# Attention with a position bias and two dense layers on one core: three tiles of head 1 scored ahead of head 0's last tile

## The chip, the cores and the metric

The kernel runs on one core of a Trainium2 chip. The metric is the device time of one execution in microseconds, the median of three runs.

## The reference, cut to what matters

```python
# q, k, v: (4, 8, 576, 64); 8 heads in each of 4 batches
scores = q @ k.T / 8
rel = |i - j|;  x = log1p(rel) / log1p(max(i, 1))
bias = relu(x * w1 + b1) @ w2            # (576, 576, 8): one table for each head, the same in all batches
attn = softmax(scores + bias);  o = attn @ v
x = o as (2304, 512)
x = (s * relu(x @ w_in)**2 + b) @ w_out  # 512 -> 2048 -> 512
h = x @ w2_in;  out = (h - tanh(h)) @ w2_out
```

All inputs and the output are float32.

## The kernel before

The program has three stages on one core. **The bias stage** builds the bias tables in 36 packs. TensorE makes them, ScalarE and VectorE write them to the tile stage, and SyncE stores each pack to bias_flat in DRAM (line 323). A bias tile (128 rows of one head, 288 KB) is read back from there with skewed rows (sp_bias). A tile can be loaded only when the packs with its rows have landed. For the last tile of head 0 (tile 4, 64 rows, 144 KB) these are all 36 (load_bias, called at line 986).

**The attention stage** runs over 32 heads (head n = batch times 8 plus head) of five row tiles each, so step g is tile t of head n with g = 5n + t. Every engine has its own function for a step, and walks through the same steps g in order. In a step, TensorE scores tile g (pe_score: four matmuls into ps_s or ps_o), VectorE adds the bias and takes the row maximum (line 767), ScalarE takes the exponential and the row sum (line 643). Five steps later, the tile of the head before is turned on TensorE (five transposes, pe_turn), rounded by ScalarE (pth, line 659), its low part is made by VectorE (ptl, line 735), and TensorE multiplies it with v (pe_value). So all matmuls have a high and a low part. The first turn of a head waits for the exponentials of all its tiles (line 590). In steps 5 to 9 the turns of head 0 thus stand beside the scores of head 1.

q and k of a head are rounded on the way: ScalarE rounds q (act_round_q, line 198), GpSimd (POOL) rounds k and makes both low parts (lines 203, 212 and 208). SyncE issues every load in the order of the steps: after VectorE's add of tile t of head n comes bias tile t of head n + 1 (line 798), and with it k (t = 2) and q (t = 4) of head n + 2.

**The dense stage** is 5 units of 64 blocks of matmuls. After 49 steps of attention alone, the other steps of attention are placed between its blocks. Its first two weight blocks are rounded by ScalarE and their low parts made by POOL after step 3 (lines 1032 and 1014).

The order is written out by hand: it is that of the loops at the end, and semaphores do the rest (s_done, min_done, exp_done and others count tiles in the order in which their engine does them).

Of the kernel before, what the change touches and what calls it, by code (L numbers as in the profile page):

```python
# [12 lines left out]
P = 128  # L13
DMA = 16
# [6 lines left out]
HIDS = 2  # L21
LATE = 2
EXTRA = 3
TURNED = 10
PLANE = 2.0 ** -15
RING = 4
# [4 lines left out]
def build(nc, qt, kt, vt, net, w2s, psi, lam, lam_rows, sb, w1, w2, w3, w4, out):  # L31
# [41 lines left out]
    def scoring(n):  # L73

        return n < BH
# [9 lines left out]
    with ExitStack() as ctx:  # L85
# [108 lines left out]

        def act_round_q(act, n):
            act.wait_ge(q_loaded, (n + 1) * DMA)
            need(act, s_done, (n - 1) * NT)
            act.activation(q2[:, n % 2, 0:S], q_raw[:], ACT.Copy, scale=lower[:, 0:1]).then_inc(q_hi_done, 1)  # L198

        def pool_round_k(pool, n):  # L200
            pool.wait_ge(k_loaded, (n + 1) * DMA)
            need(pool, s_done, (n - 1) * NT)
            pool.tensor_copy(k2h[:, n % 2, :], k_raw[:]).then_inc(k_hi_done, 1)

        def pool_low_q(pool, n):
# [18 lines left out]
            pass  # L224
        planes = tile("planes", [P, 2, 2 * S], F16)
        o_tmp = tile("o_tmp", [D, 2, HALF])
        neg_max = tile("neg_max", [P, NT])
        den = tile("den", [P, 2, NT])
        den_e = tile("den_e", [P, NT])
        inv = tile("inv", [P, NT])  # L230
# [205 lines left out]
        def slot(i):  # L436

            return i % 2

        def score_bank(n, t):  # L440

            if n == 0 and t % 2:
                return ps_o
            return ps_t if n > TURNED and (n * NT + t) % 2 else ps_s

        FIRST_PLANE = TURNED * NT
# [119 lines left out]
        def pe_score(pe, n, t):  # L566
            if t == 0:
                pe.wait_ge(q_lo_done, n + 1)
                pe.wait_ge(k_lo_done, n + 1)
            if n == 0:  # L570
                need(pe, min_done, t - 1)
                pe.wait_ge(back_done, PACKS - 2 if t == 0 else PACKS)
            elif n <= TURNED:
                pe.wait_ge(min_done, n * NT + t)
            else:
                if n == TURNED + 1 and t == 0:
                    pe.wait_ge(pt_lo_done, FIRST_PLANE)
                pe.wait_ge(p_lo_done, n * NT + t - FIRST_PLANE - 1)
            for half in range(2):
                cols = slice(half * HALF, (half + 1) * HALF)  # L580
                acc = score_bank(n, t)[:, half, 0:HALF]
                lhs = q2[:, n % 2, P * t:P * (t + 1)]
                pe.matmul(acc, lhs, k2h[:, n % 2, cols], start=True, stop=False)  # L583
                mm = pe.matmul(acc, lhs, k2l[:, n % 2, cols], start=False, stop=True)  # L584
            mm.then_inc(s_done, 1)

        def pe_turn(pe, i, alone):
            v, t = divmod(i, NT)
            if t == 0:
                pe.wait_ge(exp_done, (v + 1) * NT)  # L590
            need(pe, pt_lo_done, i - alone)
            R = ROWS[t]
            acc = turn_bank(i, alone)
            for r in range(NT):
                mm = pe.transpose(acc[0:R, P * r:P * (r + 1)], p_t[:, v % 2, r, P * t:P * t + R], ident[:])
            mm.then_inc(pt_done, 1)
# [7 lines left out]
        def pe_step(pe, g, alone):  # L604

            n, t = divmod(g, NT)
            value = pe_value if (valued(g) or 0) < FIRST_PLANE else pe_value_planes
            if t == 3 and turning(n):
                pe_turn_inv(pe, n - 1)
            if scoring(n):  # L610
                pe_score(pe, n, t)
            if valued(g) is not None and t != 2:
                value(pe, valued(g))
            if turned(g) is not None:
                pe_turn(pe, turned(g), alone)
            if valued(g) is not None and t == 2:
                value(pe, valued(g))
# [9 lines left out]
        def act_plane(act, f):  # L627
# [3 lines left out]
            act.activation(halves(plane(f)[:, 0:S]), score_home(n, t), ACT.Copy, scale=inv_n[:, t:t + 1])\  # L631
                .then_inc(p_hi_done, 1)

        def act_step(act, g, alone, between=None):
            n, t = divmod(g, NT)
            i, j = turned(g), valued(g)

            def exponential():
                if t == 0:
                    need(act, den_done, min(n - 1, TURNED))  # L640
                act.wait_ge(min_done, g + 1)
                p = score_home(n, t)
                act.activation(p, p, ACT.Exp, scale=-1.0, bias=neg_max[:, t:t + 1],
                               accum_out=den[:, n % 2, t:t + 1]).then_inc(exp_done, 1)
# [8 lines left out]
            if scoring(n) and alone and t == NT - 1:  # L653
                exponential()
# [8 lines left out]
            if scoring(n) and not (alone and t == NT - 1):  # L663
                exponential()
            if n >= TURNED and between:
                between()
            if TURNED <= n < BH:
                act.wait_ge(exp_done, g + 1)
                act.activation(sum_n[:, t:t + 1], den[:, n % 2, t:t + 1], ACT.Copy, scale=PLANE, bias=1e-9 * PLANE)\
                    .then_inc(sum_done, 1)  # L670
            if t == 0 and turning(n):
                v = n - 1
                need(act, inv_done, v)
                act.wait_ge(exp_done, (v + 1) * NT)
                act.activation(den_e[:], den[:, v % 2, :], ACT.Copy, bias=1e-9).then_inc(den_done, 1)
            if t == 1 and n + 1 < BH:
                act_round_q(act, n + 1)

        def pool_step(pool, g):
# [10 lines left out]
            if t == 1 and n >= 2 and n % 2 == 1 and n - 2 < TURNED:  # L690
                pool_scale(pool, n - 2)
                if n == H + 1:
                    pool_split(pool, KD - 1)
            if t == 1 and n + 1 < BH:
                pool_low_q(pool, n + 1)
            if t == 3 and scoring(n):
                pool.wait_ge(v_loaded, (n + 1) * DMA)
# [45 lines left out]
        def dve_plane(dve, f):  # L743
# [3 lines left out]
                                     in1=halves(plane(f)[:, 0:S]), op0=ALU.mult, op1=ALU.subtract)\  # L747
                .then_inc(p_lo_done, 1)

        def dve_step(dve, g, alone, between=None):  # L750
# [5 lines left out]
            if scoring(n):  # L756
                dve.wait_ge(s_done, g + 1)
# [5 lines left out]
            if scoring(n):  # L763
                dve.wait_ge(bias_loaded[t], (n + 1) * DMA)
                if t == 0 and n < TURNED:
                    need(dve, pt_done, (n - 1) * NT)
                dve.tensor_tensor_reduce(out=score_home(n, t), in0=score_bank(n, t)[:, :, 0:HALF],  # L767
                                         in1=halves(bias_t[:, t, :]), scale=-SCALE, scalar=3.0e38,
                                         op0=ALU.add, op1=ALU.min, accum_out=neg_max[:, t:t + 1])\
                    .then_inc(min_done, 1)  # L770
            if f is not None:
                dve_plane(dve, f)
            if i is not None:
# [16 lines left out]
        def sp_step(sp, g):  # L790
# [3 lines left out]
                sp.wait_ge(inv_row_done, v + 1)  # L794
                sp.dma_start(inv_rows[v, :].rearrange("(t p) -> t p", p=P), inv_row[:]).then_inc(inv_stored, DMA)
            if n + 1 < BH:
                sp.wait_ge(min_done, n * NT + t + 1)
                sp_bias(sp, n + 1, t)
            f = planes_of(g)
            if f is not None:  # L800
# [182 lines left out]
        @block.sync  # L983
        def _(sp):
            sp_biases(sp)
            load_bias(sp, NT - 1)
            for g in STEPS_AT[:FIRST]:
                sp_step(sp, g)
                n, t = divmod(g, NT)
                if t == 2 and n in (3, 5, 7):  # L990
                    sp_weights(sp, (n - 1) // 2)
# [35 lines left out]
        def _(act):  # L1027
            act_biases(act)
            act.wait_ge(sb_loaded, DMA)
            for g in STEPS_AT[:FIRST]:  # L1030
                act_step(act, g, True)
                if g == 3:
                    act_weights(act, 0)
                    act_weights(act, 1)
                if g == H * NT:
                    act_weights(act, 2)
# [7 lines left out]
        def _(dve):  # L1044
            dve_biases(dve)
            dve.wait_ge(sb_loaded, DMA)
            for g in STEPS_AT[:FIRST]:
                dve_step(dve, g, True)
            dve_low(dve, turned(FIRST - 1), True)
            for u in range(NU):  # L1050
# [6 lines left out]
        def _(pe):  # L1057
            pe_biases(pe)
            pe.wait_ge(ident_done, 1)
            pe.wait_ge(q_clear, 2)  # L1060
            for g in STEPS_AT[:FIRST]:
                pe_step(pe, g, True)
            pe.wait_ge(pt_lo_done, turned(FIRST - 1))
            for u in range(NU):
# [67 lines left out]
```

## Time and profile before

| | us |
|---|---|
| median of 3 runs | 1096.89 (1096.28 to 1096.93) |
| the profiled execution | 1097.03 |
| its span | 1095.2 |
| TensorE busy | 1049.5 |
| ScalarE busy | 728.6 |
| POOL busy | 681.7 |
| VectorE busy | 619.1 |

The span runs from the first to the last instruction of the program on the core; the rest of the time lies outside it. TensorE (PE in the rows, PEld for its weight loads) is busy for 96% of the span. DVE is VectorE, ACT is ScalarE, SP is SyncE and SPq its queue of transfers. The busy time of matmuls is modelled, and rows of neighbouring instructions overlap a little.

### The profile page before, as it was taken

Reading aid. Unit: us, or ns where it says so; the run is one execution under the profiler, and the core shown is the slowest. Engines: PE = TensorE matmul, PEld = TensorE weight load, DVE = VectorE, ACT = ScalarE, POOL = GpSimd, SP = SyncE. Lnnn points to the kernel's source line nnn. Section 1 sums busy time; section 2 is a strip of 40 time slices with the busy share of each in tenths; the row PEclk is TensorE's granted clock in tenths of the full one; section 3 lists DMA queues with packets and bytes.
Section 4 is the critical chain, followed back from the end, with each engine's and each line's share of the span. In section 5 each row is a group of like instructions: output and inputs, shape, how many; then the busy total and the mean of one; then the engine's idle time right before and its main releaser. Section 6 shows DMA issues by size and latency. Waiting matters only on the chain.

```text
span 1095.2 us, 16840 instructions
## 1 busy us (share of the span) xinstructions
PE 1049.5 (96%) x5668; PEld 910.9 (83%) x5668; DVE 619.1 (57%) x1128; ACT 728.6 (67%) x1469; POOL 681.7 (62%) x656
## 2 busy tenths in 40 slices
PE   5679999999999999999999999999999999999998
PEld 1158889888888888888888888888888888999998
DVE  7968877745765476567646754761450461450640
ACT  8968878866877677778767876873562563553652
POOL 1045675687778678777786787765554555455453
PEclk9989999999999999999999999999999999999999
DMA  5778876798889788998896799664333233333331
GB/s 177 256 242 273 269 225 173 194 253 239 189 218 258 215 188 234 240 214 207 242 268 169 185 255 270 171 160 131 113 98 114 96 115 124 111 129 99 97 122 63
DMA packets 185480, 202.48 MB, mean 185 GB/s; under 512 B 125954, under 2 KB 128692, under 8 KB 185396
## 3 DMA queue, kind: packets, MB, share of 16 engines
q1 hardware_dynamic: 185108, 201.35, 66.7%
q8 instruction: 45, 0.74, 0.3%
q14 instruction: 39, 0.32, 0.1%
q10 hardware_dynamic: 288, 0.07, 0.0%
HBM read 156.55 MB, written 15.64 MB: 157 GB/s over the span
## 4 chain that ended last, share of the span: by engine, by line
PE 70%; ACT 10%; issue 6%; POOL 5%; DMA 4%; DVE 4%; SPq 1%; DVEq 0%; ACTq 0%; POOLq 0%
PE ps_f L906 20%; PE ps_f L908 20%; PE ps_f L907 20%; PE ps_o L544 2%; POOL wl L863 2%; ACT x_raw L342 2%; DVE g_buf L966 2%; PE ps_s L583 2%; ACT gh L919 2%; PE ps_o L547 2%; PE ps_s L584 1%; DMA bias_flat<-stage 1%; ACT stage L359 1%; POOL pth L689 1%; ACT planes L631 1%
## 5 line engine op out<-in xcount | busy, mean ns | idle before, releaser
L863 POOL TENSOR_TENSOR wl<-w_raw,wh 128x512 fp32r<-128x512 f32 x318 | 417.5, 1318 | 282.6 <-ACT wh L856 282.1
L906 PE MATMUL ps_f<-gh,wh 128*128 128x464 f32 (+1 forms) x640 | 242.6, 379 | 1.7 <-DVE g_buf L966 1.7
L906 PE MATMUL ps_f<-xh,wh 128*128 128x464 f32 (+1 forms) x640 | 240.5, 376 | 0.6 <-DVE ptl L735 0.6
L908 PE MATMUL ps_f<-xh,wl 128*128 128x464 f32 (+1 forms) x640 | 237.4, 371 | 0.0
L907 PE MATMUL ps_f<-gl,wh 128*128 128x464 f32 (+1 forms) x640 | 237.4, 371 | 0.0
L908 PE MATMUL ps_f<-gh,wl 128*128 128x464 f32 (+1 forms) x640 | 237.2, 371 | 0.0
L907 PE MATMUL ps_f<-xl,wh 128*128 128x464 f32 (+1 forms) x640 | 237.1, 371 | 0.0
L856 ACT ACTIVATE wh<-w_raw 128x512 fp32r<-128x512 f32 x318 | 196.4, 623 | 48.8 <-PE ps_f L908 48.6
L906 PEld LDWEIGHTS ps_f<-gh,wh 128*128 128x128 f32 x640 | 120.8, 189 | 14.9 <-DVE g_buf L966 2.8
L906 PEld LDWEIGHTS ps_f<-xh,wh 128*128 128x128 f32 x640 | 120.5, 188 | 13.4 <-DVE ptl L735 0.8
L908 PEld LDWEIGHTS ps_f<-xh,wl 128*128 128x128 f32 x640 | 120.1, 188 | 13.4
L908 PEld LDWEIGHTS ps_f<-gh,wl 128*128 128x128 f32 x640 | 120.1, 188 | 13.0
L907 PEld LDWEIGHTS ps_f<-xl,wh 128*128 128x128 f32 x640 | 120.2, 188 | 12.8
L907 PEld LDWEIGHTS ps_f<-gl,wh 128*128 128x128 f32 x640 | 120.2, 188 | 11.8
L929 ACT ACTIVATE r_buf<-ps_f 128x464 f32<-128x464 f32 (+1 forms) x160 | 88.1, 551 | 58.9 <-PE ps_f L908 58.1
L957 DVE TENSOR_TENSOR gl<-g_buf,gh 128x464 fp32r<-128x464 f32 (+1 forms) x80 | 81.3, 1016 | 47.6 <-ACT gh L923 47.6
L954 DVE SCALAR_TENSOR_TENSOR gl<-g_buf,sb_c,gh 128x464 fp32r<-128x464 f32 (+1 forms) x80 | 73.8, 922 | 53.0 <-ACT gh L919 53.0
L966 DVE SCALAR_TENSOR_TENSOR g_buf<-ps_f,sb_c,r_buf 128x464 f32<-128x464 f32 (+1 forms) x80 | 55.4, 693 | 41.8 <-ACT r_buf L929 40.4
L689 POOL CAST pth<-p_t 128x576 fp32r<-128x576 f16 x110 | 77.7, 706 | 0.0
L208 POOL TENSOR_TENSOR q<-q_raw,q 128x576 fp32r<-128x576 f32 x32 | 45.8, 1432 | 44.8 <-ACT q L198 42.3
L583 PE MATMUL ps_s<-k2h,q 128*128 128x288 f32 x210 | 65.3, 325 | 6.5 <-DVE neg_max L767 6.1
L919 ACT ACTIVATE gh<-g_buf,sb_c 128x464 fp32r<-128x464 f32 (+1 forms) x80 | 54.3, 678 | 21.0 <-DVE g_buf L966 21.0
(124 smaller groups left out, 1688.7 us busy)
## 6 DMA issues: line engine op xcount, KB each, us to landing
w_raw<-in_w_out SPq DMA_DIRECT2D x80, 512.0 KB, 3.7
w_raw<-in_w_in SPq DMA_DIRECT2D x79, 512.0 KB, 3.5
bias_t<-bias_flat SPq DMA_DIRECT2D x128, 288.0 KB, 4.0
bias_flat<-stage SPq DMA_DIRECT2D x36, 295.5 KB, 2.3
k_raw<-in_kt SPq DMA_DIRECT2D x32, 288.0 KB, 4.2
q_raw<-in_qt SPq DMA_DIRECT2D x32, 288.0 KB, 3.3
v_raw<-in_vt SPq DMA_DIRECT2D x32, 288.0 KB, 3.4
bias_t<-bias_flat SPq DMA_DIRECT2D x32, 144.0 KB, 3.9
```

Of the source, the lines that this page charges most:

```text
L583: pe.matmul(acc, lhs, k2h[:, n % 2, cols], start=True, stop=False)
L689: pool.tensor_copy(pth[:, slot(i), :], turned_planes(i // NT)[:, i % NT, :]).then_inc(block_cast, 1)
L856: act.activation(wh[:, b % RING, :, :], raw_block(b), ACT.Copy)\
L863: pool.tensor_tensor(wl[:, b % RING, :, :], raw_block(b), wh[:, b % RING, :, :].bitcast(F32), ALU.subtract).then_inc(w_lo_done, 1)
L906: pe.matmul(acc, hi, rhs_h[:, k0 + kk, 0:T], start=(first and kk == 0), stop=False)
L907: pe.matmul(acc, hi, rhs_l[:, k0 + kk, 0:T], start=False, stop=False)
L908: mm = pe.matmul(acc, lo, rhs_h[:, k0 + kk, 0:T], start=False, stop=(last and kk == 3))
L919: act.activation(gh[:, j, 0:T], g_buf[:, n % 2, 0:T], ACT.Identity, bias=sb_c[:, 1:2])\
L929: act.activation(r_buf[:, n % 2, 0:T], acc, (ACT.Relu, ACT.Tanh)[l]).then_inc(r_done, 1)
L954: dve.scalar_tensor_tensor(out=gl[:, j, 0:T], in0=g_buf[:, n % 2, 0:T], scalar=sb_c[:, 1:2], in1=hi, op0=ALU.add, op1=ALU.subtract).then_i ...
L957: dve.tensor_tensor(gl[:, j, 0:T], g_buf[:, n % 2, 0:T], hi, ALU.subtract)\
L966: dve.scalar_tensor_tensor(out=g_buf[:, n % 2, 0:T], in0=acc, scalar=sb_c[:, 0:1], in1=r, op0=ALU.mult, op1=ALU.mult).then_inc(g_done, 1)
```

## The change

Three tiles of head 1 (PRE = 3, steps 5 to 7) are scored, biased and exponentiated ahead of the last tile of head 0 (step 4). Their steps keep the other work. scored_ahead(g) is the place of tile g in the new order, all_scored(n) the number of tiles scored when head n is complete. The score banks go on to alternate between ps_s and ps_o through the eight tiles. SyncE issues the last bias load of head 0 after its steps 0 to 2. ScalarE rounds q of head 1 right behind the bias stage, before the first exponential, and POOL makes its low part in step 0. The rounding of the first two weight blocks on ScalarE comes after step 4, no longer after step 3. The row maxima have two sets, for even and odd heads.

```diff
+PRE = 3
 def act_round_q(act, n):
     act.wait_ge(q_loaded, (n + 1) * DMA)
-    need(act, s_done, (n - 1) * NT)
+    need(act, s_done, all_scored(n - 2) if n > 1 else 0)
...
-neg_max = tile("neg_max", [P, NT])
+neg_max = tile("neg_max", [P, 2, NT])
...
+def scored_ahead(g):
+    if NT <= g < NT + PRE:
+        return g - 1
+    return NT + PRE - 1 if g == NT - 1 else g
+def all_scored(n):
+    return NT + PRE if n == 0 else (n + 1) * NT
+def scoring_at(g):
+    return g < TILES and not NT <= g < NT + PRE
 def score_bank(n, t):
-    if n == 0 and t % 2:
-        return ps_o
+    if n * NT + t < NT + PRE:
+        return ps_o if scored_ahead(n * NT + t) % 2 else ps_s
...
 # pe_score
-if n == 0:
-    need(pe, min_done, t - 1)
+if n * NT + t < NT + PRE:
+    need(pe, min_done, scored_ahead(n * NT + t) - 1)
...
 # pe_turn, first tile of head v
-pe.wait_ge(exp_done, (v + 1) * NT)
+pe.wait_ge(exp_done, all_scored(v))
...
 # act_step
-if t == 1 and n + 1 < BH:
+if t == 1 and 0 < n < BH - 1:
     act_round_q(act, n + 1)
 # pool_step
-if t == 1 and n + 1 < BH:
+if t == (1 if n else 0) and n + 1 < BH:
     pool_low_q(pool, n + 1)
 # sp_step
-sp.wait_ge(min_done, n * NT + t + 1)
+sp.wait_ge(min_done, scored_ahead(g) + 1)
 sp_bias(sp, n + 1, t)
...
 # SyncE
-load_bias(sp, NT - 1)
 for g in STEPS_AT[:FIRST]:
+    if g == PRE:
+        load_bias(sp, NT - 1)
     sp_step(sp, g)
...
 # ScalarE
+act_round_q(act, 1)
 for g in STEPS_AT[:FIRST]:
+    if g == NT - 1:
+        for pre in range(NT, NT + PRE):
+            act_exp(act, pre)
     act_step(act, g, True)
-    if g == 3:
+    if g == NT - 1:
         act_weights(act, 0)
         act_weights(act, 1)
...
 # VectorE, before step NT - 1
+        for pre in range(NT, NT + PRE):
+            dve_add(dve, pre)
 # TensorE, before step NT - 1
+        for pre in range(NT, NT + PRE):
+            pe_score(pe, *divmod(pre, NT))
```

act_exp and dve_add are the exponential and the add of one tile, with the lines that act_step and dve_step held before.

On SyncE, at the end of the bias stage, before (bias_flat<-stage are the last two stores, the 64-row load is head 0's last tile, the three of 128 rows are head 1's):

```order
L323 DMA bias_flat<-stage 128x591 [waits back_done] x2
L218 DMA bias_t<-bias_flat 64x576 [waits stage_stored3,stage_stored2,bias_clear,stage_stored1,stage_stored0]
L218 DMA bias_t<-bias_flat 128x576 [waits min_done] x3
L188 DMA k_raw<-in_kt 128x576 [waits k_lo_done]
L218 DMA bias_t<-bias_flat 128x576 [waits min_done]
```

and now:

```order
L324 DMA bias_flat<-stage 128x591 [waits back_done] x2
L219 DMA bias_t<-bias_flat 128x576 [waits min_done] x3
L189 DMA k_raw<-in_kt 128x576 [waits k_lo_done]
L219 DMA bias_t<-bias_flat 64x576 [waits stage_stored3,stage_stored2,bias_clear,stage_stored1,stage_stored0]
L219 DMA bias_t<-bias_flat 128x576 [waits min_done]
```

The three loads of head 1 and k of head 2 moved ahead of head 0's last tile and its wait for the stores.

On ScalarE, from the end of the bias stage to the turned tile 0 of head 0 (p_t,den is an exponential, q a rounding of q, wh one of a weight block), before:

```order
L643 ACTIVATE p_t,den<-p_t,neg_max 128x576 [waits min_done]
L198 ACTIVATE q<-q_raw,lower 128x576 [waits q_loaded]
L643 ACTIVATE p_t,den<-p_t,neg_max 128x576 [waits min_done] x2
L856 ACTIVATE wh<-r_buf 128x512 [waits w_first]
L856 ACTIVATE wh<-g_buf 128x512 [waits w_first]
L643 ACTIVATE p_t,den<-p_t,neg_max 128x576 [waits min_done]
L659 ACTIVATE pth<-ps_f 128x576 [waits pt_done]
```

and now:

```order
L199 ACTIVATE q<-q_raw,lower 128x576 [waits q_loaded,sb_loaded]
L655 ACTIVATE p_t,den<-p_t,neg_max 128x576 [waits min_done] x8
L876 ACTIVATE wh<-r_buf 128x512 [waits w_first]
L876 ACTIVATE wh<-g_buf 128x512 [waits w_first]
L674 ACTIVATE pth<-ps_f 128x576 [waits pt_done]
```

The rounding of q moved to the front, eight exponentials stand in a row, and the two weight roundings stand between the last of them and the turned tile.

## Rows read from the trace of the kernel before

**Rows 1.** The page: busy time, share of the span, instructions of each engine.

```profile
PE 1049.5 (96%) x5668; PEld 910.9 (83%) x5668; DVE 619.1 (57%) x1128; ACT 728.6 (67%) x1469; POOL 681.7 (62%) x656
```

**Rows 2.** The chain that ended last, 64 to 71.6 us: start us, us, what.

```profile
61.15 5.21 DMA bias_flat<-stage
...
66.49 2.92 DMA bias_t<-bias_flat
...
69.54 0.76 DVE p_t L767
```

**Rows 3.** Timeline of TensorE: start us, us, instruction, count, idle before it.

```profile
70.45 0.58 PE L583 MATMUL ps_s<-k2h,q 128*128 128x288 f32 x1 [6.15 <-DVE neg_max L767]
...
75.73 0.71 PE L595 MATMUL ps_f<-ident,p_t 128*128 128x128 f32 x5
...
76.86 0.38 PE L583 MATMUL ps_s<-k2h,q 128*128 128x288 f32 x1
...
80.45 0.38 PE L583 MATMUL ps_s<-k2h,q 128*128 128x288 f32 x1
```

**Rows 4.** Stretches: length, busy by engine, granted clock, DMA share, GB/s.

```profile
67.00:68.00 1.00, 0.00 (x0) 0.00 (x0) 0.00 (x0) 0.00 (x0) 1.00 (x2) 1.00 0.22 35
68.00:69.00 1.00, 0.00 (x0) 0.00 (x0) 0.00 (x0) 0.00 (x0) 1.00 (x2) 0.82 0.81 228
69.00:70.00 1.00, 0.00 (x0) 0.00 (x0) 0.46 (x1) 0.00 (x0) 0.60 (x1) 0.50 0.98 350
75.00:76.00 1.00, 1.00 (x8) 1.00 (x8) 0.58 (x3) 0.96 (x2) 1.00 (x1) 0.77 0.73 207
```

**Rows 5.** Timeline of ScalarE.

```profile
61.88 0.78 ACT L643 ACTIVATE p_t<-p_t,neg_max 128x576 f32<-128x576 f32 x1 [1.74 <-DVE neg_max L767]
...
66.29 0.61 ACT L856 ACTIVATE wh<-g_buf 128x512 fp32r<-128x512 f32 x1
...
71.02 0.18 ACT L643 ACTIVATION_READ_ACCUMULATOR p_t<-p_t,neg_max 128x1 f32 x1
72.86 0.65 ACT L659 ACTIVATE pth<-ps_f 128x576 fp32r<-128x576 f32 x1 [1.65 <-PE ps_f L595]
```

**Rows 6.** Timeline of VectorE.

```profile
61.70 0.09 DVE L767 DVE_READ_ACCUMULATOR2_ANT neg_max<- 128x1 f32 x1
...
63.37 0.08 DVE L767 DVE_READ_ACCUMULATOR2_ANT neg_max<- 128x1 f32 x1
...
74.66 0.75 DVE L735 TENSOR_TENSOR ptl<-ps_f,pth 128x576 fp32r<-128x576 f32 x1
```

**Rows 7.** Timeline of SyncE's queue: first issue, us, count.

```profile
66.49 2.09 SPq L218 DMA_DIRECT2D bias_t<-bias_flat  x4
...
70.83 0.58 SPq L183 DMA_DIRECT2D q_raw<-in_qt  x1
```

**Rows 8.** DMA view, 64 to 67.5 us: 40 slices; packets, MB, share; issues, landing.

```profile
GB/s 0 0 0 0 0 0 0 27 0 0 27 0 0 27 0 27 27 27 27 27 0 0 0 0 0 0 0 0 0 0 0 0 0 0 0 0 0 0 0 0
...
q1 hardware_dynamic: 9, 0.02, 2.1%
...
bias_t<-bias_flat SPq DMA_DIRECT2D x1, 288.0 KB, 3.1
```

**Rows 9.** DMA view, 61 to 67 us: packets, MB, share of 16 engines.

```profile
q8 instruction: 1, 0.02, 1.9%
```

**Rows 10.** DMA view, 62 to 63 us.

```profile
DMA packets 195, 0.42 MB, mean 420 GB/s; under 512 B 23, under 2 KB 23, under 8 KB 194
```

**Rows 11.** Timeline of POOL.

```profile
67.12 1.26 POOL L863 TENSOR_TENSOR wl<-r_buf,wh 128x512 fp32r<-128x512 f32 x1
...
73.99 0.66 POOL L203 CAST k2h<-k_raw 128x576 fp32r<-128x576 f32 x1 [4.38 <-DMA k_raw<-in_kt]
74.73 1.42 POOL L212 TENSOR_TENSOR k2l<-k_raw,k2h 128x576 fp32r<-128x576 f32 x1
77.20 1.43 POOL L208 TENSOR_TENSOR q<-q_raw,q 128x576 fp32r<-128x576 f32 x1 [1.04 <-ACT q L198]
```

More of the change, by code:

```diff
@@ L201, in pool_round_k @@
             pool.wait_ge(k_loaded, (n + 1) * DMA)
-            need(pool, s_done, (n - 1) * NT)
+            need(pool, s_done, all_scored(n - 2) if n > 1 else 0)
             pool.tensor_copy(k2h[:, n % 2, :], k_raw[:]).then_inc(k_hi_done, 1)
@@ L569, in pe_score @@
                 pe.wait_ge(k_lo_done, n + 1)
-            if n == 0:
-                need(pe, min_done, t - 1)
-                pe.wait_ge(back_done, PACKS - 2 if t == 0 else PACKS)
+            if n * NT + t < NT + PRE:
+                need(pe, min_done, scored_ahead(n * NT + t) - 1)
+                pe.wait_ge(back_done, PACKS - 2 if n + t == 0 else PACKS)
             elif n <= TURNED:
@@ L609, in pe_step @@
                 pe_turn_inv(pe, n - 1)
-            if scoring(n):
+            if scoring_at(g):
                 pe_score(pe, n, t)
@@ L632, in act_plane, with act_exp @@
                 .then_inc(p_hi_done, 1)
+        def act_exp(act, g):
+            n, t = divmod(g, NT)
+            if t == 0:
+                need(act, den_done, min(n - 1, TURNED))
+            act.wait_ge(min_done, scored_ahead(g) + 1)
+            p = score_home(n, t)
+            act.activation(p, p, ACT.Exp, scale=-1.0, bias=neg_max[:, n % 2, t:t + 1],
+                           accum_out=den[:, n % 2, t:t + 1]).then_inc(exp_done, 1)
         def act_step(act, g, alone, between=None):
@@ L636, in act_step @@
             i, j = turned(g), valued(g)
[L638 to L644, printed above, removed]
             if j is not None and j % NT == NT - 1:
@@ L652, in act_step @@
                 act_plane(act, f)
-            if scoring(n) and alone and t == NT - 1:
-                exponential()
+            if scoring_at(g) and alone and t == NT - 1:
+                act_exp(act, g)
             if i is not None:
@@ L662, in act_step @@
                 between()
-            if scoring(n) and not (alone and t == NT - 1):
-                exponential()
+            if scoring_at(g) and not (alone and t == NT - 1):
+                act_exp(act, g)
             if n >= TURNED and between:
@@ L673, in act_step @@
                 need(act, inv_done, v)
-                act.wait_ge(exp_done, (v + 1) * NT)
+                act.wait_ge(exp_done, all_scored(v))
                 act.activation(den_e[:], den[:, v % 2, :], ACT.Copy, bias=1e-9).then_inc(den_done, 1)
-            if t == 1 and n + 1 < BH:
+            if t == 1 and 0 < n < BH - 1:
                 act_round_q(act, n + 1)
@@ L748, in dve_plane, with dve_add @@
                 .then_inc(p_lo_done, 1)
+        def dve_add(dve, g):
+            n, t = divmod(g, NT)
+            dve.wait_ge(s_done, scored_ahead(g) + 1)
+            dve.wait_ge(bias_loaded[t], (n + 1) * DMA)
+            if t == 0 and n < TURNED:
+                need(dve, pt_done, (n - 1) * NT)
+            dve.tensor_tensor_reduce(out=score_home(n, t), in0=score_bank(n, t)[:, :, 0:HALF],
+                                     in1=halves(bias_t[:, t, :]), scale=-SCALE, scalar=3.0e38,
+                                     op0=ALU.add, op1=ALU.min, accum_out=neg_max[:, n % 2, t:t + 1])\
+                .then_inc(min_done, 1)
         def dve_step(dve, g, alone, between=None):
@@ L755, in dve_step @@
                 dve_scale(dve, f)
-            if scoring(n):
-                dve.wait_ge(s_done, g + 1)
+            if scoring_at(g):
+                dve.wait_ge(s_done, scored_ahead(g) + 1)
             if t == 3 and turning(n):
@@ L762, in dve_step @@
                 dve.tensor_copy(inv_row[:], ps_s[0:NT, 0, HALF:HALF + P]).then_inc(inv_row_done, 1)
[L763 to L770, printed above, removed]
+            if scoring_at(g):
+                dve_add(dve, g)
             if f is not None:
@@ L1047, in _ @@
             for g in STEPS_AT[:FIRST]:
+                if g == NT - 1:
+                    for pre in range(NT, NT + PRE):
+                        dve_add(dve, pre)
                 dve_step(dve, g, True)
@@ L1061, in _ @@
             for g in STEPS_AT[:FIRST]:
+                if g == NT - 1:
+                    for pre in range(NT, NT + PRE):
+                        pe_score(pe, *divmod(pre, NT))
                 pe_step(pe, g, True)
```

## The prediction

> **What bounds the kernel now.** I read the page first. TensorE is busy for 1049.5 us of the 1095.2 us span [rows 1], so a change can only take from what lies around its work: idle time of TensorE, or work done at the low clock. Then the chain of waits between the bias stage and head 1, the place the change touches. There the end hangs on transfers: the last store to bias_flat is issued at 61.15 and takes 5.21 us, then head 0's last bias tile is loaded in 2.92 us, and only at 69.54 can VectorE add it [rows 2]. The TensorE timeline shows the price: it has nothing to do for 6.15 us until 70.45 [rows 3]. The stretches show a second price: the granted clock is 0.82 in 68 to 69, 0.50 in 69 to 70 and 0.77 in 75 to 76 [rows 4]. So it fell to the 1.2 GHz level at about 68.64, 4.4 us after TensorE stopped, and came back to 2.4 GHz at about 75.46, some 5 us after work resumed. From 70.45 on, TensorE works at half speed: scores of head 1 between the turns of head 0.
>
> **The change part by part.**
>
> *Three scored tiles move out of the way.* They run before the last tile of head 0, whose bias tile holds everything. I compare the start of the score of head 1's tile 3, the first that stands where it stood: 76.86 [rows 3]. I follow what precedes it after the change, first with the load of head 0's last tile landing when it does now. ScalarE's exponential of that tile ends at 71.02 + 0.18 = 71.20 [rows 5]. Then ScalarE has the two weight roundings, which the change moves from before the gap to here: 0.61 us each by the row [rows 5], about 1.0 for both since neighbouring rows on this engine overlap by 0.1. TensorE meanwhile turns tiles 0 and 1 (at full clock the first is done well before 72.2). ScalarE's rounding of turned tile 0 takes 0.65 [rows 5]: 71.2 + 1.0 + 0.65 = 72.85. VectorE's low part, 0.75 [rows 6]: 73.6. Then TensorE turns tile 2, makes the first value product and turns the inverses: now 75.73 to 76.86, that is 1.13 at full clock [rows 3]. Together 73.6 + 1.13 = 74.75, against 76.86: 2.1 us earlier, call it 2.05 with the wake-ups. The three scores in the gap cost nothing: TensorE is idle there. Behind that point each step holds what it held.
>
> *The clock.* The sum assumes 2.4 GHz in the turns. After the change TensorE has four scores after 63.5 instead of one; two of them wait for adds of tiles whose bias lands at about 65 to 67.5, so its pauses come to some 2 to 3 us each instead of one of 6.15. The only fall in the work came 4.4 us into a pause, and I expect none. The Trainium skill (TensorE: Matmul & The Clock Gate, Part 1) says that the activity window is "free-running", so where a fall lands would differ from run to run; the row above agrees with a fall in a pause, and the trace of before can't show the phase. Sparse work in the gap could then still lose the clock, which is a rival below.
>
> *The transfers that now go first.* SP used to stand at the wait for the last store until 66.49 and then issued four bias loads in a row [rows 7]. Now it issues three loads of head 1 as soon as the adds of head 0's tiles 0 to 2 are through (61.79 for tile 0, 63.45 for tile 2 [rows 6]) and k of head 2, four of 288 KB, all ahead of the tile that matters. From 64 to 67.5 the DMA engines are all but empty: 9 packets [rows 8]. So mostly the loads fill a hole. But why is the last store late? In 61 to 67 one instruction-fetch packet took 1.9% of 16 engines over 6 us, which is 1.8 us of one engine [rows 9], and the nine packets left after 64 (2.1% of 16 x 3.5 us = 1.2 us of one engine, ending near 65.8 by the GB/s slices) are that one engine's share of the store [rows 8]. TensorE's code is the same up to there, so I expect the fetch and the late store again. Behind it on this engine stand its sixteenths of four loads. At the full rate of 420 GB/s [rows 10] 295 KB take 0.70 us, four 2.8: that engine is free for head 0's last tile at 68.6. Its bytes now start at about 67.8 (a DMA share of 0.22 in 67 to 68 [rows 4]). So the landing moves by 0 (if the held engine catches up) to 0.8 us; the far end is below. I take 0.5, nearer to 0.8 than to nothing.
> The Trainium skill (DMA: Bandwidth & Descriptors, Queues, rings and completion order) has the rule behind this: on each of the 16 engines descriptors are taken in ring order, and each engine adds its own increment. By that rule the delay is the 0.8, without it 0; the trace agrees as far as the one engine's late share of the store goes.
>
> *q of head 1 rounded at the stage's end.* ScalarE's 0.77 leaves the row of exponentials and goes into a wait of 1.74 before the first of them [rows 5]; POOL's low part of q, 1.43 by the same operation for head 2 [rows 11], is ready at about 62.3, before TensorE wants it at 63.5. Nothing.
>
> *The rest.* The weight roundings start about 5.5 us later, so POOL's two low parts of 1.26 start at 71.8 instead of 67.12 [rows 11], and head 2's k (0.66 + 1.42) and q (1.43) stand behind them: with 0.5 of delay 72.3 + 2.5 + 2.1 + 1.4 = 78.3. TensorE wants them for head 2's first score, now at 80.45 [rows 3], then at about 78.9. Hidden with 0.6 to spare; if the cover is gone, each us late costs one. Head 2's k now waits 4.38 for its load [rows 11], and will not. q of head 2 is still issued behind the last add (now 70.83 [rows 7], then 71.3); it needs to land by about 75.5, and the queue ahead of it is shorter than now. The maxima per parity cost nothing: same sizes. The added waits on SP (the last bias load behind k of head 2) hold nothing that was issued earlier before.
>
> Sum: 2.05 - 0.5 = 1.55 us. The profiled execution took 1097.03 with the span 1095.2; it gives 1095.5. The median is 0.14 lower, so 1095.4.
>
> **The rivals.**
> *The last tile is not late, or the store is not held (22%).* For it: a hole of 3.5 us stands open for loads. Then the gain is 2.05 (1094.9); were the store down with the engines that had no fetch, some 2.2 us sooner, 4.2 in all: 1092.7. Against it: the fetch goes with the code, which is unchanged.
> *The clock falls (11%).* Then turn 0 ends 0.4 later than ScalarE is free for it and 1.13 becomes 2.26: 1.5 lost, the gain is nothing, 1096.9. If it stays low for 6.8 us, as it does now, from the turns at 71.8 to 78.6, another 1.8 us of work at half speed lose 0.9: 1097.8. Against it: no pause as long as 4.4.
> *Slower: head 1's loads stand in front in full (7%).* If the hole is not used, since the four loads only begin to move when the store is down, head 0's last tile comes behind them. The row for head 1's first tile, issued into an empty queue, has 3.1 us [rows 8]; a k load issued behind four bias loads has its rounding only at 73.99 [rows 11]. Head 0's tile would then land near 72.9 instead of 69.4: 3.4 lost against 2.05 won, 1098.3. It decides against the change from a landing after 71.4. Against it: only one of 16 engines is held.
> *The gain is given back (8%)* in heads 1 to 8, where TensorE pauses for short waits on x, q and transfers: 1096.5.
>
> **How the numbers follow.** The forecast has 52%, for 1095.4, with its own range 1094.3 to 1096.4. About 0.2% (2.2 us) is what a measurement of this kernel can tell from no change. A gain of more than that, under 1094.7: 0.10 of the forecast's 0.52 and 0.14 of the first rival's 0.22, with 0.01 of the rest: 0.25. A loss of more, over 1099.1: 0.03 from the loads, 0.02 from the clock: 0.05. Within: 0.70. The range takes in the forecast, the clock's 1097.8 on one side and half way into the early store on the other: 1093.4 to 1097.8.
>
> **What would show it.** In the changed kernel TensorE has four scores between 63.5 and about 69.5, three of them head 1's; no row of granted clock under 1.00 between 60 and 90; VectorE's add of head 0's last tile at about 70.0 (69.54 now); the last store again 5.2 us with a fetch beside it; the score of head 1's tile 3 at about 75.3 (76.86 now); head 2's first score at about 78.9 without a wait for POOL. I am wrong if that add comes after 71.4, if the clock falls, or if the 1.5 us at head 1 are gone by the time the weight blocks start.

## The result, and the profile after

| | before | after |
|---|---|---|
| median, runs | 1096.91 us, 10 | 1099.95 us, 10 |
| lowest to highest | 1095.92 to 1098.78 | 1097.51 to 1101.36 |
| the profiled execution, its span | 1097.03, 1095.2 | 1097.51, 1095.6 |

The ratio is 1.0022 with the interval 1.0014 to 1.0030: slower, by a little over the 0.2% that can be told here. I had expected 1095.4. Runs of either kernel differ by 3 to 4 us, for the most part since TensorE's clock is low for a longer or shorter time (within the four sets of runs below, time and mean clock of the kernel before go together with a correlation of -0.74 to -0.87). Each run lists its mean clock, and I use it below. Of the 132 later runs of the kernel before, five of 1294 to 5822 us are left out as disturbed, and in means and in the fit also one with a mean clock of 0.946.

The chain of waits of the changed kernel, 58 to 90 us (start us, us, what), which answers to [rows 2]:

```profile
61.28 5.38 DMA bias_flat<-stage
66.80 3.57 DMA bias_t<-bias_flat
70.53 0.76 DVE p_t L771
71.33 0.88 ACT p_t L655 x2
72.25 1.34 PE ps_f L610 x5
73.62 0.66 ACT pth L674
74.30 0.77 DVE ptl L750
75.11 1.33 PE ps_f L610 x5
```

The order did what it says: the last store is again held for over 5 us, and after the add ScalarE goes on to the weights while TensorE turns. But the add stands at 70.53, not at 70.0, and the first group of five turns takes 1.33 us, against 0.71 for such a group at 78.17, when the clock is up again. TensorE's timeline, with [rows 3]:

```profile
68.30 0.40 PE L598 MATMUL ps_s<-k2h,q 128*128 128x288 f32 x1 [2.69 <-DVE neg_max L771]
...
72.25 1.33 PE L610 MATMUL ps_f<-ident,p_t 128*128 128x128 f32 x5 [2.40 <-ACT p_t L655]
...
77.02 0.38 PE L598 MATMUL ps_s<-k2h,q 128*128 128x288 f32 x1
```

The pause of 6.15 has become two, of 2.69 and 2.40, as forecast. The last row is the score of head 1's tile 3: 77.02, where it stood at 76.86 [rows 3] and I had it at 75.3. The stretches of the changed kernel (columns as in [rows 4]) say why:

```profile
69.00:70.00 1.00, 0.85 (x5) 0.56 (x4) 0.77 (x2) 0.97 (x5) 0.00 (x0) 0.94 0.71 237
70.00:71.00 1.00, 0.00 (x0) 0.00 (x0) 0.47 (x1) 0.81 (x2) 0.00 (x0) 0.50 0.03 12
...
76.00:77.00 1.00, 1.00 (x8) 0.96 (x7) 0.12 (x1) 0.00 (x0) 1.00 (x1) 0.65 0.98 360
```

The granted clock fell to the 1.2 GHz level at 69.88 and came back at 76.71, as long as before (6.83 us) and 1.2 us later. It fell just as TensorE stopped for the second time, after a pause of 2.69 and 1.6 us of work: no pause of over 4 us was needed.

What follows the place is slower too. Start of VectorE's output operation for heads 0 to 3, of the kernel before:

```profile
84.59 0.75 DVE L784 SCALAR_TENSOR_TENSOR x_raw<-ps_o,o_tmp 64x576 f32<-64x576 f32 x1
93.90 0.75 DVE L784 SCALAR_TENSOR_TENSOR x_raw<-ps_o,o_tmp 64x576 f32<-64x576 f32 x1 [0.15 <-ACT o_tmp L648]
103.36 0.75 DVE L784 SCALAR_TENSOR_TENSOR x_raw<-ps_o,o_tmp 64x576 f32<-64x576 f32 x1 [0.15 <-ACT o_tmp L648]
112.69 0.75 DVE L784 SCALAR_TENSOR_TENSOR x_raw<-ps_o,o_tmp 64x576 f32<-64x576 f32 x1
```

and of the changed one:

```profile
84.84 0.75 DVE L804 SCALAR_TENSOR_TENSOR x_raw<-ps_o,o_tmp 64x576 f32<-64x576 f32 x1
94.66 0.75 DVE L804 SCALAR_TENSOR_TENSOR x_raw<-ps_o,o_tmp 64x576 f32<-64x576 f32 x1
104.22 0.75 DVE L804 SCALAR_TENSOR_TENSOR x_raw<-ps_o,o_tmp 64x576 f32<-64x576 f32 x1
113.67 0.75 DVE L804 SCALAR_TENSOR_TENSOR x_raw<-ps_o,o_tmp 64x576 f32<-64x576 f32 x1
```

Heads were 9.31, 9.46 and 9.33 us apart and are 9.82, 9.56 and 9.45 apart, where the order of the instructions is the same. What waits there, on VectorE from 76 to 158 us (us in total, times, longest), before:

```profile
DVE p_t L767 <- PE ps_s L584: 5.4, 16, 0.8
```

and after:

```profile
DVE p_t L771 <- PE ps_s L599: 7.5, 23, 0.7
```

Seven more of the adds count as waiting for their score. One add of head 0, which has nothing else to wait for, in the changed kernel:

```profile
62.24 0.76 DVE L771 CUSTOM_DVE_ANT_0 p_t<-ps_o,bias_t 128x576 f32<-128x576 f32 x1 [0.32 <-PE ps_o L599]
```

It starts 0.94 after its score began (61.30). Before, the same add started 0.84 after its score (61.17):

```profile
62.01 0.76 DVE L767 CUSTOM_DVE_ANT_0 p_t<-ps_o,bias_t 128x576 f32<-128x576 f32 x1 [0.22 <-PE ps_o L584]
```

The code says what differs, and the section on the change has it wrong: dve_add does not hold just the lines that dve_step held. The add moved into a function that waits for the score itself, and the step that calls it kept its own wait. VectorE waits for s_done twice ahead of each add but the three early ones:

```diff
 # dve_step
-if scoring(n):
-    dve.wait_ge(s_done, g + 1)
+if scoring_at(g):
+    dve.wait_ge(s_done, scored_ahead(g) + 1)
 ...
-    dve.wait_ge(bias_loaded[t], (n + 1) * DMA)
-    dve.tensor_tensor_reduce(...)
+    dve_add(dve, g)
+# dve_add
+    dve.wait_ge(s_done, scored_ahead(g) + 1)
+    dve.wait_ge(bias_loaded[t], (n + 1) * DMA)
+    dve.tensor_tensor_reduce(...)
```

### The profile page after: what moved, and what is told of

Same layout as the page of the kernel before. It is cut to its first block, busy times and chain, and to the rows that moved or that the text cites. A ratio compares the mean times of both kernels' runs of the same rounds, so it can differ in the third digit from the quotient of the medians.

```text
span 1095.6 us, 16862 instructions
## 1 busy us (share of the span) xinstructions
PE 1050.8 (96%) x5668; PEld 910.7 (83%) x5668; DVE 620.6 (57%) x1128; ACT 729.1 (67%) x1469; POOL 681.9 (62%) x656
## 4 chain that ended last, share of the span: by engine, by line
PE 73%; ACT 10%; issue 6%; POOL 5%; DVE 4%; DMA 1%; DVEq 0%; SPq 0%; ACTq 0%; POOLq 0%
PE ps_f L926 20%; PE ps_f L928 20%; PE ps_f L927 20%; ACT x_raw L343 2%; POOL wl L883 2%; PE ps_o L559 2%; PE ps_s L598 2%; DVE g_buf L986 2%; PE ps_s L599 2%; ACT gh L939 2%; PE ps_o L562 2%; PE ps_o L574 1%; POOL pth L704 1%; ACT planes L646 1%; ACT stage L360 1%
## 5 line engine op out<-in xcount | busy, mean ns | idle before, releaser
L559 PE MATMUL ps_o<-pth,vhl 128*128 128x288 f32 x220 | 60.9, 341 | 6.1 <-POOL pth L704 5.1
```

The source lines that it names most:

```text
L559: mm = pe.matmul(ps_o[:, half, 0:HALF], vhl[:, n % 2, u, :], pth[:, slot(i), cols], start=(u == 0), stop=(u == NT - 1))
```

## The experiments

They ran in four sets, each on a chip of its own and with its own runs of the kernel before: 1 to 3; 4 to 6; 7 and 8; 9. Single numbers are medians. Ratios are against the kernel before of the same set, and "in its set" compares means there.

### 1. The changed kernel again

The kernel as it is.

> The changed kernel once more. Its ten runs showed mean granted clocks of 0.997 (1097.5 us), 0.994 (some 1099.1) and 0.992 (1098.3 to 1099.5 us of span), and the one profile was of the rarest kind, 0.997. Theory 1 (clock): a profile of the common kind shows low clock for 13 to 17 us instead of 6.8, beginning in the gap of 65 to 72 us, and the time is 1099 to 1101. Rival (the path): the late landing of head 0's last tile (its add at 70.53 instead of 69.54) and the two weight roundings behind it cost the time, and the low clock is only a companion; then the profile differs from the one in hand by more than TensorE's rate, in waits for transfers.

Measured: 1098.63 us (12 runs), ratio 1.0013 (1.0003 to 1.0023). The clock was low for 6.83 us from 69.27. Slower again, by less than the first time. The profile was once more of the rare kind, 0.997, so it doesn't test the first theory. The profile of 3 does, at 0.992: it shows 17.1 us of low clock, 10.2 of them in the gap.

### 2. The pauses filled, in either kernel

In the changed kernel, 20 transposes of the identity after the second early score and 16 after head 0's last score; their result is never read.

```diff
+def pe_fill(pe, count):
+    for i in range(count):
+        pe.transpose(flat(ps_t)[:, 0:P], ident[:], ident[:])
 ...
 for pre in range(NT, NT + PRE):
     pe_score(pe, *divmod(pre, NT))
+    if pre == NT + 1:
+        pe_fill(pe, 20)
 pe_step(pe, g, True)
+if g == NT - 1:
+    pe_fill(pe, 16)
```

> The changed kernel with 20 transposes of the identity on TensorE after the second of head 1's early scores and 16 after the score of head 0's last tile, written to ps_t where nothing else is; they fill some 2 us each of TensorE's two pauses. Theory 1 (clock): the clock stays at 1.00, the score of head 1's tile 3 starts near 76 and the time is 1095.5 to 1096.5, that is 3 to 4 us under the changed kernel. Rival (the path): the clock is no cause; the time stays within 0.7 us of the changed kernel's 1099.95, or is longer by what of the filling runs over.

Measured: 1098.40 (12 runs), 1.0005 (0.9994 to 1.0015). That is not the 3 to 4 us under the changed kernel that were expected: in its set it is 1.1 under it (1097.98 against 1099.07). In the kernel before, 50 of them:

```diff
 pe_step(pe, g, True)
+if g == NT - 1:
+    pe_fill(pe, 50)
```

> The kernel before with 50 transposes of the identity on TensorE after the score of head 0's last tile, some 5.5 us in its pause of 6.15 us. Theory 1 (clock): the granted clock stays at 1.00 and the turns and scores from 70.45 to 75.46 run at full speed: some 1.5 to 2.5 us under the kernel before, 1094.4 to 1095.4. Rival (the chain of turned tile, rounding and low part sets the pace there, whatever the clock): within 0.5 us of the kernel before.

Measured: 1096.95 (11 runs), 0.9997 (0.9988 to 1.0006), 0.5 us under the kernel before in its set, where 1.5 to 2.5 were expected. Two stretches of the changed kernel with the pauses filled:

```profile
69.00:70.00 1.00, 1.00 (x10) 1.00 (x10) 0.74 (x2) 0.85 (x3) 0.00 (x0) 1.00 0.77 254
75.00:76.00 1.00, 1.00 (x10) 0.96 (x9) 0.32 (x1) 0.78 (x1) 0.94 (x2) 1.00 0.95 325
```

The clock stays up there in both. The score of head 1's tile 3 comes at 75.81 against 77.02, so the low clock costs 1.2 us at this place. But with the pauses filled in both, the changed kernel is still the slower by the means of the set (1097.98 against 1097.01, with a standard error of 0.6), and its first heads are still 9.83 us apart: something else holds it up. By the few runs at the full clock throughout it isn't slower (1096.26, five runs, against 1096.37, four).

### 3. k of head 2 loaded behind head 0's last tile

```diff
 # sp_step
-if t == 2 and n + 2 < BH:
+if t == 2 and 0 < n < BH - 2:
     load_k(sp, n + 2)
 # SyncE
 if g == PRE:
     load_bias(sp, NT - 1)
+    load_k(sp, 2)
```

> The changed kernel with the load of head 2's k behind head 0's last bias tile instead of ahead of it, so three loads of 288 KB stand in front instead of four. Theory 2 (queue): the landing of that tile was delayed by the loads ahead of it on the one DMA engine that the instruction fetch holds; a quarter of them less gives 0.2 to 0.7 us back at its add (70.53), and as much of the time if the clock lets it. Rival: the landing is set by the last store alone (5.38 us) and the add stays at 70.5; time unchanged.

Measured: 1099.36 (11 runs), 1.0017 (1.0008 to 1.0025); no gain. In its profile the loads in front took longer by themselves (head 1's first bias tile 6.18 us), the second early score was late, and the add of head 0's last tile, at 72.12, waited for its score and no more for its load:

```profile
72.12 0.76 DVE L771 CUSTOM_DVE_ANT_0 p_t<-ps_o,bias_t 128x576 f32<-128x576 f32 x1 [0.29 <-PE ps_o L599]
```

The load itself took 2.7 us, as in the old order, but the last store took 6.2 us, so the loads in front had longer to land. The run doesn't decide what delays the load.

### 4. The second wait taken out, and put into the kernel before

```diff
-def dve_add(dve, g):
+def dve_add(dve, g, waited=False):
-    dve.wait_ge(s_done, scored_ahead(g) + 1)
+    if not waited:
+        dve.wait_ge(s_done, scored_ahead(g) + 1)
 # dve_step
-    dve_add(dve, g)
+    dve_add(dve, g, True)
```

> The changed kernel, but the add of a tile on VectorE waits for its score once, as before, not twice (moving the add into a function of its own left one wait in the step and put a second into the function). Theory 3 (second wait): with the second wait VectorE's add starts 0.93 us after the score's first matmul instead of 0.84, and heads 1 to 8 are 9.46 to 9.82 us apart instead of 9.32 to 9.46; with one wait the spacing is that of before and the time falls by 0.6 to 1.1 us, to about 1098.5 over all clocks. Rival (transfers or the lost clock make the heads slower): spacing and time stay as they are in the changed kernel (mean of 22 runs 1099.4).

Measured: 1098.14 (11 runs), 0.9999 (0.9988 to 1.0010). The other way round, in the kernel before:

```diff
 if scoring(n):
+    dve.wait_ge(s_done, g + 1)
     dve.wait_ge(bias_loaded[t], (n + 1) * DMA)
```

> The kernel before with the wait for the score repeated ahead of VectorE's add, and nothing else. Theory 3: heads 1 to 8 are 9.45 us or more apart, 0.1 to 0.15 more than before each, and the time is 0.6 to 1.1 us over the kernel before (mean of 35 runs 1097.5). Rival: a wait that is already met costs nothing, time and spacing as before within 0.3 us.

Measured: 1098.54 (12 runs), 1.0007 (0.9998 to 1.0017), 0.8 us above the kernel before in its set. By the ratio alone that is not certain; the traces are clear. Its add of head 0 starts 0.93 after its score (61.05), with an idle time of 0.31 for 0.22:

```profile
61.98 0.76 DVE L768 CUSTOM_DVE_ANT_0 p_t<-ps_o,bias_t 128x576 f32<-128x576 f32 x1 [0.31 <-PE ps_o L584]
```

The output operations of heads 0 to 2 show it too. With the second wait taken out of the changed kernel:

```profile
86.27 0.75 DVE L805 SCALAR_TENSOR_TENSOR x_raw<-ps_o,o_tmp 64x576 f32<-64x576 f32 x1
95.61 0.75 DVE L805 SCALAR_TENSOR_TENSOR x_raw<-ps_o,o_tmp 64x576 f32<-64x576 f32 x1 [0.16 <-ACT o_tmp L663]
105.07 0.75 DVE L805 SCALAR_TENSOR_TENSOR x_raw<-ps_o,o_tmp 64x576 f32<-64x576 f32 x1
```

and with a second wait in the kernel before:

```profile
84.94 0.75 DVE L785 SCALAR_TENSOR_TENSOR x_raw<-ps_o,o_tmp 64x576 f32<-64x576 f32 x1
94.78 0.75 DVE L785 SCALAR_TENSOR_TENSOR x_raw<-ps_o,o_tmp 64x576 f32<-64x576 f32 x1
104.33 0.75 DVE L785 SCALAR_TENSOR_TENSOR x_raw<-ps_o,o_tmp 64x576 f32<-64x576 f32 x1
```

9.34 and 9.46 without, 9.84 and 9.55 with it, whatever the order of the scores. In all profiles heads 0 and 1 are 9.31 to 9.34 apart with one wait (12 profiles) and 9.82 to 9.84 with two (five). The longer spacing goes with the wait. And without it the changed kernel can't be told from the one before: the early scores by themselves bring nothing that shows as long as the clock falls.

### 5. One wait and filled pauses

The edits of 2 (in the changed kernel) and 4 together.

> The changed kernel with one wait and with the transposes of the identity in TensorE's two pauses. Theories 1 and 3 together (clock and second wait): no low clock between 60 and 90 us, heads spaced as before, 1095.3 to 1096.3 and so 1.2 to 2.2 us under the kernel before. Rival (what is gained ahead of head 1 is given back in heads 1 to 8 by transfers, whatever the waits): 1097 to 1098, with TensorE waiting for q of a head (0.91 us at 119 in the filled kernel) and for x.

Measured: 1096.44 (12 runs), 0.9982 (0.9973 to 0.9991), 1.6 us under the kernel before in its set, with no low clock in the gap and the first heads 9.33 us apart.

### 6. Only one tile ahead

`PRE = 1`, with one wait.

> The changed kernel with one wait and only one tile of head 1 ahead of head 0's last (PRE = 1). Theory 1 (clock) in its second half: the clock comes back late in the changed kernel since TensorE has only turns, with pauses, after 72 us; with two scores back among the turns it works without pause and the mean clock goes from 0.9937 to the 0.9953 of before. Time 1097 to 1097.8. Rival: the clock is lost in the gap alone, whatever stands behind it; mean clock 0.994 or lower, time 1098.4 or more.

Measured: 1097.40 (11 runs), 0.9994 (0.9984 to 1.0005), 0.4 us under the kernel before in its set; too little to tell.

### 7. Repeats

The kernel before with 50 transposes, and one wait with filled pauses:

> The kernel before with the filled pause, again, beside the next two for the same chip. With a full clock behind the gap it shows what the changed order is worth without the clock in play. All theories: 1096.2 to 1097.2, that is 0.3 to 1.0 us under the kernel before.

> The changed kernel with one wait and filled pauses, again. Theory A (the early scores are worth what was forecast once the clock holds and the second wait is gone): 1.0 to 1.6 us under the kernel before with the filled pause. Rival (they are worth nothing, and the 1096.4 of the first time was the chip's): within 0.4 us of it.

Measured: 1096.39, 0.9987 (0.9976 to 0.9999), and 1096.50, 0.9984 (0.9972 to 0.9997), 12 runs each. Between the two lie 0.3 us (means), not the 1.0 to 1.6 of theory A. One wait alone:

> The changed kernel with one wait and no filling, again, for a closer interval and for its clocks. Theory 1 (clock): mean clock 0.994, below the kernel before's own in the same call by about 0.001, and a time 1 to 2 us over one_wait_fill_again, so within 0.5 us of the kernel before. Rival: mean clock and time lie with one_wait_fill_again's.

Measured: 1097.36 (12 runs), 0.9997 (0.9987 to 1.0008).

### 8. Head 0's last tile on a queue of its own

The kernel of 5, with this load issued by ScalarE.

```diff
 # SyncE
-if g == PRE:
-    load_bias(sp, NT - 1)
 # ScalarE
 if g == NT - 1:
+    load_bias(act, NT - 1)
     for pre in range(NT, NT + PRE):
         act_exp(act, pre)
```

> The changed kernel with one wait and filled pauses, and the load of head 0's last bias tile issued on ScalarE's queue behind its fourth exponential, no longer on SyncE's behind the loads of head 1. Theory 2 (queue): from issue to landing it takes 2.8 to 3.0 us as in the kernel before, not the 3.6 to 3.9 of the changed one; the add of that tile comes 0.5 to 0.9 us earlier and the time falls by 0.3 to 0.8 us under one_wait_fill_again. Rival (the DMA engines are simply shared by more bytes, in whatever queue): landing and time as in one_wait_fill_again.

Measured: 1097.45 (12 runs), 0.9993 (0.9983 to 1.0003), 1.1 us above the kernel of 5 in its set. From its chain, 58 to 90 us:

```profile
66.43 4.69 DMA bias_t<-bias_flat
```

and its DMA view, 61 to 72 us (queue, packets, MB, share; issues, KB, us to landing):

```profile
q10 hardware_dynamic: 80, 0.15, 4.9%
...
bias_t<-bias_flat ACTq DMA_DIRECT2D x1, 144.0 KB, 4.7
```

On SP's queue the same load took 3.75 us in the kernel of 5 (repeat). Not behind the others in their queue, it took longer, not shorter. But the edit did one thing more. SyncE no longer stands at the wait for the stores, so it issued the fourth bias tile of head 1 at 65.45, ahead of head 0's last tile (66.43):

```profile
65.45 7.11 SPq L219 DMA_DIRECT2D bias_t<-bias_flat  x2
```

In the kernel of 5 (repeat) that load comes behind it. So a longer row of loads went first here, and the run doesn't test the queue alone. The Trainium skill (DMA: Bandwidth & Descriptors, Issuing engines are not separate DMA queues) says that all queues run on the same 16 engines; the trace agrees as far as a queue of its own made the load no quicker.

### 9. A third time, and one tile ahead with filled pauses

> The kernel before with the filled pause, a third time, as the base for the next two on one chip: 1096.4 to 1097.2.

> The changed kernel with one wait and filled pauses, a third time. Theory B (with a full clock the early scores are worth nothing, since in the trace head 0's output is ready 22.1 us after the first add, against 21.9 in the kernel before with the filled pause): within 0.4 us of before_fill_third. Theory A (they are worth a part of what was forecast): 0.5 to 1.3 us under it. So far 24 and 23 runs differ by 0.43 us with a standard error of 0.37.

Measured: 1097.48, 0.9998 (0.9988 to 1.0008), and 1095.76, 0.9987 (0.9979 to 0.9996), 11 runs each; the second is 1.3 us under the first (means), for theory A and against B. The filled pauses don't hold the clock always. In this profile of the second kernel it fell behind them, at the third group of turns, for 3.4 us:

```profile
73.00:74.00 1.00, 0.70 (x7) 0.46 (x5) 0.06 (x1) 1.00 (x4) 1.00 (x1) 1.00 0.88 207
...
75.00:76.00 1.00, 1.00 (x6) 1.00 (x6) 0.43 (x1) 0.74 (x1) 1.00 (x2) 0.50 0.96 336
```

TensorE still waits there for 1.21 us ahead of its first turns and for 1.06 behind the second.

Then `PRE = 1`, one wait, and 44 transposes after head 0's last score:

> The changed kernel with one wait, one tile of head 1 ahead (PRE = 1) and 44 transposes of the identity in TensorE's pause. Theory B: the number of tiles ahead doesn't matter, time within 0.4 us of the other two. Rival: the three loads ahead of head 0's last bias tile delay it (issue to landing 3.6 to 3.9 us instead of 2.9), and with one load ahead fewer of them do; then this is the best of the three, 0.4 us or more under one_wait_fill_third.

Measured: 1095.21 (11 runs), 0.9978 (0.9969 to 0.9986): faster than both kernels, 2.3 us under the one before in its set. It is 0.6 under three tiles ahead (means, standard error 0.4), which doesn't settle that one tile is the better number. Its chain, 58 to 90 us:

```profile
61.54 5.43 DMA bias_flat<-stage
67.11 2.85 DMA bias_t<-bias_flat
70.09 0.76 DVE p_t L777
```

and two of its stretches:

```profile
69.00:70.00 1.00, 1.00 (x12) 1.00 (x11) 0.00 (x0) 0.44 (x2) 0.00 (x0) 1.00 0.84 240
...
74.00:75.00 1.00, 1.00 (x7) 0.89 (x8) 0.88 (x3) 1.00 (x3) 1.00 (x2) 1.00 0.97 309
```

With two loads fewer in front, head 0's last tile takes 2.85 us, about as it did before (2.92 [rows 2]). In 6 it took 3.00.

### The runs put together

Means over the runs with their standard errors, and the mean over those that had the full clock throughout (1.000 in the run's list):

| | runs | mean us | mean clock | at clock 1.000 |
|---|---|---|---|---|
| before (1 to 9) | 126 | 1097.83 ± 0.12 | 0.995 | none |
| before, two waits | 12 | 1098.79 ± 0.27 | 0.995 | none |
| changed, two waits (first comparison, 1) | 22 | 1099.38 ± 0.31 | 0.994 | none |
| changed, one wait (4, 7) | 23 | 1097.82 ± 0.24 | 0.994 | none |
| one tile ahead, one wait (6) | 11 | 1097.55 ± 0.35 | 0.995 | none |
| before, filled (2, 7, 9) | 34 | 1096.93 ± 0.22 | 0.998 | 1095.82 (10) |
| changed, two waits, filled (2) | 12 | 1097.98 ± 0.5 | 0.998 | 1096.26 (5) |
| changed, one wait, filled (5, 7, 9) | 35 | 1096.21 ± 0.18 | 0.998 | 1095.11 (12) |
| one tile ahead, one wait, filled (9) | 11 | 1095.13 ± 0.35 | 1.000 | 1094.79 (9) |

No run without filled pauses has more than 0.997. That is 6.83 us at the half clock (6.83 / 2 / 1095 = 0.003), the stretch in the gap. All eight profiles without filled pauses have it, in either order; of the nine with filled pauses one has a fall there. The mean clock of the kernel before is 0.9949 and that of one wait 0.9944, as in the kernel before of its sets. Two waits have 0.9937, so a part of the changed kernel's loss in these means is clock; why it loses more of it, no run tells. With the mean clock as a term of the fit described at the end, the second wait costs 1.1 us in either order (standard error 0.3), and 1.7 between the two filled kernels with three tiles ahead.

## Why the prediction was wrong

**The clock ("I expect none") failed.** It fell at 69.88 (0.94 in the stretch 69 to 70 above, 0.50 in the next), and the turns took 1.33 us for five. I had read one fall, 4.3 us into a pause (64.30 to 68.64), as if a long pause were what it takes. The rival had priced it: the gain is nothing. That is what one wait shows, 0.9999 and 0.9997. At this place the low clock costs 1.2 us (77.02 against 75.81).

**The sum was right for the full clock, and counted the clock's share as the order's.** I had the score of head 1's tile 3 5.2 us after the add of head 0's last tile (69.54 to 74.75). With filled pauses and the clock up it is 5.25 (after_fill, 70.56 to 75.81) and 5.24 (one wait filled, 70.51 to 75.75). But the 7.32 us of before (69.54 to 76.86 [rows 2, 3]) hold the low clock: in the kernel before with filled pauses it is 6.02 (69.87 to 75.89). So of the 2.05 us, 1.30 were clock and 0.78 order. In the changed kernel as it is, low clock on both sides, it is 6.49: 0.83 won.

**The delay of head 0's last tile: 1.0 us, not 0.5.** Its load takes 3.57 for 2.92 us, its issue comes 0.31 later (66.80 for 66.49), and the add is at 70.53 for 69.54. In other profiles with three tiles and k in front and on the same queue the load took 3.54 to 4.17. From the issue of the last store to the add it is 7.72 to 8.39 us in four profiles of the old order, 8.98 to 9.46 in seven with three tiles ahead, and 7.99 and 8.55 with one. So the delay is no accident of one profile, and it is above my bound of 0.8. It grows with what is loaded in front, but my reason for it, the order in the one held engine, is not shown: the queue of its own (8) had one load more in front, and with k behind (3) the load took 2.7 but its add waited for a late score. Which engine's share comes last, the profile doesn't say.
At this place 0.83 us are won and 0.99 lost: 76.86 becomes 77.02.

**"Behind that point each step holds what it held" failed.** The second wait on s_done makes each add start about 0.1 us later after its score; I had taken the add to be the one that the step held before, and read over the line. With it the changed kernel is slower: 1.1 us at the full clock (1096.26 against 1095.11, from different sets), 1.6 in the means without filling (1099.38 against 1097.82), of which 0.4 is the mean clock. Putting it into the kernel before costs 1.0 by the pooled means and 0.8 in its set. The rival "given back in heads 1 to 8" named the place by chance; its cause, x, q and transfers, was another.

Together: 1095.4 with 1.2 for the clock, 0.5 for the delay and 1.1 for the wait is 1098.2. The repeat gave 1098.63. The first comparison gave 1099.95; six of its ten runs had a mean clock of 0.992, which means some 10 us more of low clock than in its profile (0.997).

**Right:** the last store, held again with a fetch beside it (5.38 us); four scores in the gap and its pauses; q of head 1; the work of POOL. Its weight parts start at 72.80 and q of head 2 ends at 78.78, half a us later than I had it, and head 2's first score comes at 80.68 (80.45 before [rows 3]) without a wait for it.

**Open.** What the early scores bring at the full clock. Pooled it is 0.7 us (1095.82 against 1095.11; over all filled runs 0.72 ± 0.28). But four of the ten runs behind 1095.82, with a mean of 1096.37, are from a set without the one-wait kernel. In the two sets that have both it is 0.54 (four against five runs) and 0.04 (two against four), and over all their runs 0.3 and 1.3. By the account above 0.78 won and about 1 lost should leave nothing. One tile ahead has 0.32 us less from the add to the score of tile 3 (5.70 for 6.02). At the full clock it is 1.0 us faster than the pooled kernel before (1094.79 against 1095.82), but 0.36 faster than the two such runs in its own set. How its 2.3 us over the kernel before divide between clock and order, these runs don't settle. What comes after the place is larger than such differences: from the output operation of head 0 to that of head 7 the same kernel (one wait, filled) took 68.4 us in one profile and 66.2 in two.

## What to carry to other kernels

When a change shortens a stretch that lies at the low clock, work out both sides at the same clock: else the clock's share is counted as the order's gain, and it comes only if the clock really stays up. Splitting one pause of TensorE into two doesn't keep its clock; harmless work in the pauses did, in eight of nine profiles. When code moves into a function, list the waits of the function and of its caller side by side: a wait that is already met still cost about 0.1 us each time here, and that counts where the other engines wait for the one that has it.

## What the runs showed of the hardware

A second wait on a semaphore that has been reached costs VectorE 0.09 to 0.1 us for each add (0.94 for 0.84 us from score to add; idle 0.32 for 0.22, and 0.31 when put into the kernel before). For 160 adds that would be 15 us; about 1 us of it reaches the end, probably since VectorE is busy for only 57% of the span [rows 1] and mostly not what the others wait for.

Low clock lasted 3.4 to 10.2 us at a time, and not only in the gap: in one wait (4) the granted clock was 0.50 also for 3.4 us each from 16.33, 40.23 and 221.13. Around 221 us TensorE has work all the time, by its modelled busy rows:

```profile
221.00:222.00 1.00, 1.00 (x5) 0.87 (x4) 0.00 (x0) 0.00 (x0) 1.00 (x3) 0.57 0.81 137
...
223.00:224.00 1.00, 1.00 (x4) 0.90 (x3) 0.00 (x0) 0.00 (x0) 1.00 (x2) 0.50 1.05 324
```

3.4 us at the low clock cost about 1.0 us over all runs (627 ± 32 us for each unit of mean clock, times 0.0016, in a fit with one constant for each kernel and set), less than the 1.7 us that half of them would be. In the gap it costs less still: filled pauses raised the mean clock by 0.0035 (before) and 0.0038 (one wait), which by the fit would be 2.2 and 2.4 us, and gave 0.9 and 1.6. That part of the low clock falls into time in which TensorE waits anyway would explain both; it isn't shown. The Trainium skill (TensorE: Matmul & The Clock Gate, Part 1) calls the activity window "free-running"; that the same kernel has between one and several low stretches, and begins the one in the gap at 69.88 in one profile and at 69.27 in another, agrees with it.
